# One attention unit per step, with the queues staggered, in place of two units per step

## What is computed

```python
def _attn_ref(q, k, v, n_sink, window):      # 2 x 8 heads, 768 positions, 64 wide
    scores = scale * np.matmul(q, k.transpose(0, 1, 3, 2))
    keep = is_sink | ((rel >= 0) & (rel < int(window)))   # 4 sinks, window 128
    scores = np.where(keep, scores, -1000000000.0)
    a = np.exp(scores - np.max(scores, axis=-1, keepdims=True))
    a = a / (np.sum(a, axis=-1, keepdims=True) + 1e-09)
    return np.matmul(a, v)

def _moe_ref(x, w_gate, w_noise, noise, w1, w2):   # 1536 tokens, 8 experts
    noisy_logits = x @ w_gate + np.log1p(np.exp(x @ w_noise)) * noise
    ...  # the two best experts of each token, with softmax weights
        h = np.maximum(x[mask] @ w1[e], 0.0)
        out[mask] += top2_w[mask, k, None] * (h @ w2[e])

def _moe2_ref(x, w_in, w_out):
    h = x @ w_in
    return (h * np.tanh(np.log1p(np.exp(h)))) @ w_out
```

## Time and profile before

| | us |
|---|---|
| runs | 804.93, 807.20, 807.74 |
| median | 807.20 |
| the profiled execution's own time | 804.93 |
| its span | 803.2 |
| attention with the gates, until the last `values` | about 122 |
| routing, until the first slot's matmuls | about 122 to 141 |
| the 31 slots | about 141 to 525 |
| last layer | about 525 to 803 |

### The profile page before, as it was taken

How to read it: one execution, slowest core, us unless ns; L and a number is a source line. 1 busy time by engine, 2 the same in 40 slices (tenths; PEclk the granted TensorE clock), 3 DMA queues, 4 the chain that set the end, 5 groups by cost and what they waited for, 6 DMA issues and landing times.

```text
span 803.2 us, 13152 instructions
## 1 busy us (share of the span) xinstructions
PE 775.8 (97%) x4116; PEld 643.2 (80%) x4117; DVE 517.0 (64%) x944; ACT 278.8 (35%) x553; POOL 304.0 (38%) x307
## 2 busy tenths in 40 slices
PE   9999994999999999999999999998999999999997
PEld 6888883788888888888888888786888888888886
DVE  5686876454454454454544544558998888888776
ACT  5665652203110302003030300145555555454453
POOL 3366672929281652817337554550111010000000
PEclk9999996999999999999999999999999999999999
DMA  7689562736372451715427353120100100000001
GB/s 204 184 237 304 146 207 55 208 103 199 104 223 79 125 175 37 228 62 156 144 62 227 102 184 109 37 66 1 53 27 27 53 27 27 1 28 25 1 0 53
DMA packets 61442, 86.15 MB, mean 107 GB/s; under 512 B 30104, under 2 KB 34200, under 8 KB 61400
## 3 DMA queue, kind: packets, MB, share of 16 engines
q1 hardware_dynamic: 43400, 37.23, 15.1%
q10 hardware_dynamic: 13600, 33.96, 14.1%
q0 software_dynamic: 4400, 14.42, 6.4%
HBM read 69.35 MB, written 16.25 MB: 107 GB/s over the span
## 4 chain that ended last, share of the span: by engine, by line
PE 88%; DVE 5%; ACT 2%; SPq 1%; issue 1%; DMA 1%; another core or an unknown queue 1%; POOL 0%; DVEq 0%; ACTq 0%; POOLq 0%
PE bank L1321 21%; PE bank L1332 21%; PE bank L1393 15%; PE bank L1374 15%; PE bank L1229 4%; PE bank L1305 3%; PE bank L1182 2%; PE bank L1298 2%; PE bank L1192 1%; PE bank L1214 1%; PE bank L1232 1%; SPq L448 1%; PE bank L1167 1%; DMA k_in<-in_k 1%
## 5 line engine op out<-in xcount | busy, mean ns | idle before, releaser
L563 POOL TENSOR_TENSOR wgt<-stage,wgt 128x1024 f32 (+1 forms) x64 | 151.2, 2403 | 106.6 <-ACT wgt L738 106.6
L1332 PE MATMUL bank<-wgt,hT 128*128 (+1 forms) x744 | 185.7, 398 | 0.0
L1321 PE MATMUL bank<-wgt,xT 128*128 (+1 forms) x744 | 182.4, 394 | 1.5 <-DVE xT L1049 1.5
L1321 PEld LDWEIGHTS bank<-wgt,xT 128*128 128x128 f32 x744 | 137.3, 188 | 28.9 <-DVE xT L1049 1.7
L1332 PEld LDWEIGHTS bank<-wgt,hT 128*128 128x128 f32 x744 | 135.2, 188 | 25.8
L738 ACT ACTIVATE wgt<-stage 128x1024 f32 (+1 forms) x64 | 61.6, 1045 | 269.6 <-PE bank L1332 259.4
L1393 PE MATMUL bank<-wgt,gT 128*128 128x512 f32 x576 | 141.2, 395 | 4.9 <-DVE gT L1110 4.9
L1374 PE MATMUL bank<-x2T,wgt 128*128 128x512 f32 (+1 forms) x588 | 138.1, 385 | 0.9 <-DVE x2T L1087 0.9
L1393 PEld LDWEIGHTS bank<-wgt,gT 128*128 128x128 f32 x576 | 108.5, 190 | 28.6 <-DVE gT L1110 6.1
L1374 PEld LDWEIGHTS bank<-x2T,wgt 128*128 128x128 f32 x588 | 108.7, 188 | 23.0 <-POOL wgt L635 1.1
L1055 DVE TENSOR_SCALAR h<-bank 128x512 f32<-128x512 f32 x62 | 42.9, 691 | 63.9 <-PE bank L1321 61.8
(11 more groups left out here) (169 smaller groups left out, 963.7 us busy)
## 6 DMA issues: line engine op xcount, KB each, us to landing
stage<-in_moe_w ACTq DMA_DIRECT2D x48, 512.0 KB, 4.3
stage<-in_moe_w SPq DMA_DIRECT2D x16, 512.0 KB, 6.7
y_dram<-y_sb SPq DMA_DIRECT2D x31, 256.0 KB, 2.4
stage<-in_moe_w_in ACTq DMA_DIRECT2D x8, 512.0 KB, 4.5
stage<-in_moe_w_out ACTq DMA_DIRECT2D x8, 512.0 KB, 3.7
v_turn<-in_v_turned SPq DMA_DIRECT2D x8, 404.5 KB, 3.7
v_in<-in_v SPq DMA_DIRECT2D x8, 390.0 KB
x_dram<-x_sb SPq DMA_DIRECT2D x16, 192.0 KB, 3.2
```

Of the source, the lines that this page charges most:

```text
L563: nc.gpsimd.tensor_tensor(cols(parity, 1, u * UNIT, UNIT), stage[:, u, :], cols(parity, 0, u * UNIT, UNIT).bitcast(fp32), ALU.subtract).th ...
L1321: ins = T.matmul(HA[half][:], xT[:, a, c, :], cols(par, b, c * F + half * 512, 512), start=c == 0 and n == 0, stop=c == NC - 1 and n == 2)
L1332: ins = T.matmul(YB[kk % 2][:], hT[:, a, c, :], cols(par, b, NC * UNIT + c * DM, DM), start=c == 0 and n == 0, stop=c == F // P - 1 and n ...
```

## The change

Each pass of the loops now handles one unit per step, with the engines at different distances. PE runs S(n+2), T(n+1), V(n-1) in pass n; ACT runs `pT_step`(n+1), `exp_step`(n+2), then at most one piece of `round_qk` and one `gate_step`; DVE runs `norm_step`(n-2), `merge_step`(n+2), then at most one `qk_remainder`; POOL takes `cut_probs`(u) and then one piece of `first_set` after each unit rather than after each two. What the first pass had as exceptions now stands ahead of the loops (S(0), S(1), the first gates, T(0) on PE). In the last pass `noisy_gates` and the `pick` steps of DVE are spread over single units. SP's list is the same row for row. The loads of q and k of a pair, which ACT waited for together, are now waited for apart, each ahead of its own first piece.

```diff
@@ POOL
-            for n in range(0, NP * QT, 2):
-                cut_probs(n)
-                cut_probs(n + 1)
-                for u in (n, n + 1):
-                    if u >= WEIGHTS_FROM and (u - WEIGHTS_FROM) // 4 < UNITS and (u - WEIGHTS_FROM) % 4 < 3:
-                        first_set((u - WEIGHTS_FROM) // 4, (u - WEIGHTS_FROM) % 4)
...
+            for u in range(NP * QT):
+                cut_probs(u)
...
+                if u >= WEIGHTS_FROM and (u - WEIGHTS_FROM) // 4 < UNITS and (u - WEIGHTS_FROM) % 4 < 3:
+                    first_set((u - WEIGHTS_FROM) // 4, (u - WEIGHTS_FROM) % 4)
@@ ACT
+            exp_step(0, 0, 0)
+            exp_step(0, 0, 1)
+            for step in range(GATE_STEPS):
+                gate_step(0, 0, step, GATE_FIRST[step])
+            act.wait_ge(masks_ready, 1)
+            pT_step(0, 0, 0)
...
-                for n in range(0, 2 * QT, 2):
+                for n in range(2 * QT):
                     hp, par, t = at_unit(it, n)
-                    exp_step(hp, par, t)
-                    exp_step(hp, par, t + 1)
...
-                    pT_step(hp, par, t)
-                    pT_step(hp, par, t + 1)
-                    if not (last and par == 1):
+                    if not (last and n + 1 >= 2 * QT):
+                        pT_step(*at_unit(it, n + 1))
+                    if not (last and n + 2 >= 2 * QT):
+                        exp_step(*at_unit(it, n + 2))
+                    if t < 4 and not (last and par == 1):
                         hp1, par1, _ = at_unit(it, n + QT)
+                        if t < 2:
+                            act.wait_ge((k_loaded if t % 2 else q_loaded)[par1], 16 * (hp1 + par1))
                         if t == 0:
                             wait(act, scores_ready, QT * (2 * hp + par))
-                            act.wait_ge(q_loaded[par1], 16 * (hp1 + par1))
-                            act.wait_ge(k_loaded[par1], 16 * (hp1 + par1))
-                            round_qk(par1, 0)
-                            round_qk(par1, 1)
...
+                        round_qk(par1, t)
+                    if (n + 1) % QT >= GATE_AT and not (last and par == 1):
+                        hp1, par1, t1 = at_unit(it, n + 1 + QT)
+                        gate_step(hp1, par1, t1 - GATE_AT, GATE_OUT[t1 % 2])
@@ DVE
-                for n in range(0, 2 * QT, 2):
+                for n in range(2 * QT):
                     hp, par, t = at_unit(it, n)
-                    if not (first and n == 0):
-                        merge_step(hp, par, t)
-                        merge_step(hp, par, t + 1)
-                    for side in range(2):
-                        if not (first and n == 0):
-                            norm_step(*at_unit(it, n - 2 + side))
-                        if t > 0 and not (last and par == 1):
-                            hp1, par1, _ = at_unit(it, n + QT)
-                            qk_remainder(hp1, par1, t - 2 + side)
+                    if not (first and n < 2):
+                        norm_step(*at_unit(it, n - 2))
+                    if not (last and n + 2 >= 2 * QT):
+                        merge_step(*at_unit(it, n + 2))
+                    if 1 <= t <= 4 and not (last and par == 1):
+                        hp1, par1, _ = at_unit(it, n + QT)
+                        qk_remainder(hp1, par1, t - 1)
@@ PE
+            scores(0, 0, 0)
+            scores(0, 0, 1)
+            for step in range(GATE_STEPS):
+                gate_parts(0, step, GATE_FIRST[step])
+            turn_probs(0, 0, 0)
...
-                for n in range(0, 2 * QT, 2):
-                    hp, par, t = at_unit(it, n)
-                    final = last and n == 2 * QT - 2
-                    scores(hp, par, t)
-                    scores(hp, par, t + 1)
...
-                        values(*at_unit(it, n - 2))
-                        if not final:
-                            values(*at_unit(it, n - 1))
-                    turn_probs(hp, par, t)
-                    if first and n == 0:
+                for n in range(2 * QT):
+                    if not (last and n + 2 >= 2 * QT):
+                        scores(*at_unit(it, n + 2))
+                    if first and n < 2:
                         fill(1)
-                    if final:
+                    if not (last and n + 1 >= 2 * QT):
+                        turn_probs(*at_unit(it, n + 1))
+                    if not (first and n == 0):
                         values(*at_unit(it, n - 1))
-                    turn_probs(hp, par, t + 1)
```

More of the change, by code:

```diff
@@ L694, in _ @@
                 round_qk(0, piece)
+            exp_step(0, 0, 0)
[4 more added lines that the diff above has]
+            pT_step(0, 0, 0)
             def body(it):
                 last = isinstance(it, int) and it == NP // 2 - 1
-                first = isinstance(it, int) and it == 0
-                for n in range(0, 2 * QT, 2):
+                for n in range(2 * QT):
@@ L700, in body @@
                     hp, par, t = at_unit(it, n)
-                    exp_step(hp, par, t)
-                    exp_step(hp, par, t + 1)
-                    if first and n == 0:
-                        for step in range(GATE_STEPS):
-                            gate_step(0, 0, step, GATE_FIRST[step])
-                        act.wait_ge(masks_ready, 1)
-                    pT_step(hp, par, t)
-                    pT_step(hp, par, t + 1)
-                    if not (last and par == 1):
+                    if not (last and n + 1 >= 2 * QT):
+                        pT_step(*at_unit(it, n + 1))
@@ L724, in body @@
-                    if last and n == 2:
+                        round_qk(par1, t)
+                    if (n + 1) % QT >= GATE_AT and not (last and par == 1):
+                        hp1, par1, t1 = at_unit(it, n + 1 + QT)
+                        gate_step(hp1, par1, t1 - GATE_AT, GATE_OUT[t1 % 2])
+                    if last and n == 3:
                         softplus(0)
@@ L947, in body @@
                 first = isinstance(it, int) and it == 0
-                for n in range(0, 2 * QT, 2):
+                for n in range(2 * QT):
                     hp, par, t = at_unit(it, n)
-                    if not (first and n == 0):
-                        merge_step(hp, par, t)
-                        merge_step(hp, par, t + 1)
-                    for side in range(2):
-                        if not (first and n == 0):
-                            norm_step(*at_unit(it, n - 2 + side))
-                        if t > 0 and not (last and par == 1):
-                            hp1, par1, _ = at_unit(it, n + QT)
-                            qk_remainder(hp1, par1, t - 2 + side)
+                    if not (first and n < 2):
[5 more added lines that the diff above has]
+                        qk_remainder(hp1, par1, t - 1)
                     if last and n == 0:
                         gate_sums(0, 0, QT).then_inc(sums_ready, 1)
-                    if last and n == 4:
+                    if last and n == 5:
                         noisy_gates(0)
@@ L964, in body @@
                         pick_max(0, 0, rt3["lg"][:, 0:QT])
+                    if last and n == 7:
                         pick_first(0, 0)
@@ L968, in body @@
                         pick_max(0, 1, by_token("cut"))
+                    if last and n == 9:
                         pick_first(0, 1)
@@ L1237, in body @@
                 first = isinstance(it, int) and it == 0
-                for n in range(0, 2 * QT, 2):
-                    hp, par, t = at_unit(it, n)
-                    final = last and n == 2 * QT - 2
-                    scores(hp, par, t)
-                    scores(hp, par, t + 1)
[L1243 to L1248, removed]
-                        values(*at_unit(it, n - 2))
-                        if not final:
-                            values(*at_unit(it, n - 1))
-                    turn_probs(hp, par, t)
-                    if first and n == 0:
+                for n in range(2 * QT):
+                    if not (last and n + 2 >= 2 * QT):
+                        scores(*at_unit(it, n + 2))
+                    if first and n < 2:
                         fill(1)
-                    if final:
+                    if not (last and n + 1 >= 2 * QT):
+                        turn_probs(*at_unit(it, n + 1))
+                    if not (first and n == 0):
                         values(*at_unit(it, n - 1))
-                    turn_probs(hp, par, t + 1)
             stream_loop(pe, NP // 2, body)
-            values(NP // 2 - 1, 1, QT - 2)
             values(NP // 2 - 1, 1, QT - 1)
```

5 lines of the change are left out of this document (3 added, 2 removed).

## The result

The changed kernel takes 813.32 us (median of five runs, 812.20 to 815.35) against 807.20 for the kernel before (five runs, 804.93 to 807.74): a ratio of 1.0085, 95% interval 1.0062 to 1.0106. It is slower by 6.1 us by the medians; the forecast was 813.5. The profiled execution took 815.96, more than any of the five, with a span of 814.2.

The account below looks back on a forecast made before the run. PE was taken to bound the kernel, in attention too. Borders +10.1 us, less 3.5 us of idle time, other engines nothing: +6.6 on the 807.2 median gives 813.8; forecast 813.5, range 804 to 820.

Parts of the forecast that it names:

- The borders: PE in attention: added changes between 64-row and 128-row steps cost 0.44 us per two units, 23 times, +10.1 us.
- V to S: PE's step from V to S, shown in no row: a border adding 0.20 to 0.23 us to V's 1.17.
- T: PE's step T, now followed by V instead of S: 0.24 + 0.11 = 0.35 us.
- The idle time: PE's waits in attention, 7.4 us in all: 3.9 stay, so 3.5 us come back.
- the steady pairs: Staggering hides the 2.37 us chain from S to T under 2.87; 1.6 us left for units that are close.
- The late load: PE's wait at 70.6 us behind ACT's late load of k: 0.2 of 1.45 us left.
- The last two pairs: PE's waits where DVE runs routing pieces, 2.8 us before: 0.9 stays, at T of the last unit.
- The start: PE's waits at the second T of the program and the first V behind the fill: 1.2 us stays.
- The other engines at nothing: DVE, ACT, POOL and SP do the same operations in the new order; each costed at 0 us.
- Rival 1: PE's waits go almost wholly and borders cost their least: +3.0 us, 810.2 us; chance 0.17.
- rival 2: Faster: V to S is hidden as S's loads slip under V's last pass; 801.7 us, chance 0.09.
- Rival 3: DVE reaches the merge late, so the S-to-T chain outgrows 2.87 us in each unit; 822 us, chance 0.12.

Follow-up runs that it names:

- e4: Changed kernel with the eleven stores that fill spare rows of y_dram moved from the fifth pair's turn of SP to the eighth's; 813.15 us.
- e5: Kernel before with the eleven stores that fill spare rows of y_dram moved from the fifth pair's turn of SP to the eighth's; 805.07 us, ratio 0.9978.
- e11: Changed kernel with merge_step(n+2) put ahead of norm_step(n-2) on DVE; 812.90 us.
- e14: Kernel before with POOL's list alone in the new order, one piece behind each unit's masks; 813.23 us, ratio 1.0084.
- e7: Kernel before with PE's list alone in the new order, one unit per step; 892.81 us.
- e8: Changed kernel with PE's list alone put back to two units per step; 855.31 us in its one run.
- e9: Kernel before with a small unused matmul of 32 columns over 64 rows added ahead of each V of an odd tile; 815.35 us.
- e10: Kernel before with the same small matmul ahead of each V of an odd tile, but over 128 rows, so no added border; 809.48 us.
- e13: Changed kernel with POOL's list alone put back: masks of two units, then the pieces of first_set; 815.08 us.

## Why the prediction was right, and where only its sum was

The forecast, its direction and its main mechanism hold: PE pays for borders that were not there. But two terms were mis-sized against each other, by 2.3 and 2.8 us, and that they nearly cancel is luck. So is the last digit of the agreement, 813.5 against 813.32: the sum had +6.6 us, the stage took 7.6 more in its trace, and the medians differ by 6.1.

**The borders: +10.1 predicted, +7.8 measured.** V to S, which no row showed, is 0.366 from the last load: the upper bound, 0.14 + 0.23. A lone S is 0.57 as worked out. The term that failed is T: 0.35 predicted, 0.28 measured. I took T's first step, 0.24 between the loads at 37.55 and 37.79, from a T that stands behind V. Behind a border T's second load follows its first by 0.06 instead of 0.14. The same close step shows in the second T of the earlier trace rows, which stands behind a short wait (38.14 - 37.97 = 0.17 for both steps against 0.24); I had not compared the two. The step of two units was also read with a small wait in it, 4.17 for 4.10. So two units cost 2 x (1.37 + 0.57 + 0.28) = 4.44 against 4.10, 0.34 x 23 = 7.8.

**The idle time: -3.5 predicted, -0.7 measured.** By the starts of the loads, without the steps at borders, PE waited for 6.8 us before and 6.1 after. Part by part:

- Within the steady pairs the staggering works as argued, even better: four waits of 0.09 to 0.18 are left, where I had left 1.6, all at units behind the short V, as named. The units of tile 1 wait 0.1 at most, in four places.
- The late load: 0.2 was to be left of 1.45; it was 2.1. The prediction looked at the load that was late (k) and not at the one queued behind it on SP (v_turn), which PE needs at nearly the same moment. e4 and e5 show the stores ahead of both as the cause.
- The last two pairs: 0.9 was to be left; it was 2.8. The chain there was longer by routing pieces that lasted four to six times their length beside POOL (0.93 for 0.21, 1.16 for 0.26, 1.28 for 0.21). I had costed POOL and DVE each by its own load, not by when they meet.
- The start, 1.2 to be left, has about 0.5.

7.8 - 0.7 = 7.1, where the table has 7.6. The 0.5 between them is not placed: the table's gates and fills are shorter after the change, not longer.

**The other engines at nothing.** DVE's norm ahead of the merge costs nothing (e11). SP's list is the same, but the late load above is its work, so nothing was too low. ACT's list was not tested by itself. POOL was right for the wrong reason: its new list is worth 6.7 us against PE's old one (e14) and nothing against PE's new one, because V stands further behind.

**The rivals.** Rival 1 (the waits go) and rival 2 (V to S hidden) are refuted by the rows above. Rival 3 (the chain outgrows its cover in every unit) did not come; e7 and e8 show what that would look like. Rival 4, the clock, came in the profiled execution: its slots took 2.4 us longer than before.

**Signs.** 47 blocks of S: yes, one of 12 and 46 of 6, with 9.6 us of idle ahead of them. A unit's step of 2.3: 2.2 to 2.3. The stage's end near 128: 130. Waits of T under 2.5: no, 3.0 by the row that names the exponentials, and 1.4 under "issue". No wait at the load: the one for k did not come, the one for v_turn did. Slots and last layer: 2.4 us more in the slots, where the clock fell, and 0.1 in the last layer.

## What to carry to other kernels

Count the places where PE changes between steps over 64 and 128 rows before putting steps one by one: here each costs 0.20 to 0.23 us, and a finer interleaving that gave PE hardly any idle time back doubled their number. Read the cost of a step at every kind of neighbour that it has in the trace, its inner gaps as well: T's second load stood 0.06 behind its first at a border and 0.14 behind V. Lists of engines that hand units to one another are one schedule, and putting one of them in another order by itself can cost far more than the whole change (e7, e8, e14). e14 also suggests to put a long piece of side work where its engine's next due result is far away: 1.27 us of it between two units' masks cost 6.7 us.

## What the runs showed of the hardware that I had not expected

- The cost of a border goes with the columns of the pass ahead of it: 0.23 us behind a pass of 162 columns (e9 against e10, and after), 0.20 behind one of 128 (T to S), 0.09 behind one of 32 (e9 against e10).
- A small DVE operation with two SBUF operands that started beside a POOL subtraction lasted until POOL's ended (1.33 us for 0.20 in e13, 1.28 for 0.21 in after). A larger one, the remainder of L862 at 91.77 us in after, took 1.02 where 0.56 is usual and ended 0.43 behind POOL. The Trainium skill (GPSIMD Engine Reference, Specifications) lists contention between GpSimd and DVE instructions with two SBUF inputs; the trace agrees, and shows the small one held until the large one's end.
- The time of one kernel's executions goes with their mean granted clock. Of the twenty runs of the kernel before beside e5, the eight with a mean granted clock of 0.989 took 804.97 to 805.92 us, and the eleven with 0.985 took 806.89 to 810.20. The stretch of 6.8 us at 1.2 GHz in the first slot, above, is such a difference in one trace. Differences of 2 us between medians here can be that alone. At equal clock the change costs somewhat more than its medians say, as far as runs of different sessions can be compared: the two executions of after with 0.989 took 812.78 and 813.32, some 7 to 8 us above the eight of before, and the three with 0.985 took 813.73, 815.35 and 815.96, about 7 above the median of the eleven (808.46).
